# Feed-forward stages of an attention kernel: another order of the activations' low parts and the partial sums' copies on VectorE and ScalarE, one activation sum a step on GpSimd, last store in halves

## The chip, the cores and the metric

One core of a Trainium2 chip. The metric is the time of one execution on the device in microseconds (us), median of the runs. Engines by their short names: PE is TensorE, PEld its weight loads, DVE is VectorE, ACT is ScalarE, POOL is GpSimd, SP is SyncE (it only issues DMAs here).

## What is computed

```python
def reference(**kwargs):
    attn_out = _attn_ref(...)          # B, H, S, D = 4, 8, 576, 64: local softmax attention plus a memory read
    x = np.ascontiguousarray(attn_out.transpose(0, 2, 1, 3)).reshape(B * S, H * D)   # 2304 tokens x 512
    x = _moe_ref(x=x, **moe_kwargs)    # g = x @ w_gate; silu(g) * (x @ w_val) @ w_out      (512 -> 1536 -> 512)
    return _moe2_ref(x=x, **moe2_kwargs)   # h = x @ w_in; g = h where h >= 1, 0 where h <= -1, else (h + 1)**2 / 4; g @ w_out  (512 -> 2048 -> 512)
```

Everything is float32. The change touches only what follows the attention: the two feed-forward layers.

## The kernel before, in words

**Split numbers.** A float32 product is made of three fast matmuls: every operand is split into a high part (a copy rounded to the fast type, made by ACT) and a low part (raw minus high, made by DVE or POOL). `three` (lines 1284 to 1286) issues high x high, high x low, low x high.

**Steps.** The 2304 tokens are three superblocks (SB = 768, each held as two halves of 384 columns). Layer one takes 12 steps u for each superblock (u = 0 to 35, S1 = 12), layer two 8 steps (u = 36 to 59, S2 = 8). A step computes one tile of hidden units of the first layer or two of the second. The up projection of a step is a fast 2x2 scheme with seven products instead of eight: `product(u, n)`, n = 0 to 6, each of six matmuls of 384 columns. It needs seven forms of the activations, X0 to X6, for the superblock: four are the activations themselves or sums of them (X1, X3, X5, X6 are sums that POOL makes, `x_sum`, line 609), each with a high part by ACT (`x_high`, line 725) and a low part by DVE (`x_low`, line 972). There is one buffer for each of the seven, so the high part n of the next superblock waits until product n of the last step of this one has read it. Product n of the first step of a superblock waits for the low parts 0 to n. "Fresh" is the first step of a superblock (u = 12, 24, 36, 44, 52), "ends" the last (u = 11, 23, 35, 43, 51).

**Inside a step.** ACT copies partial sums out of PSUM: `copy_p1` (753) after product 0, `copy_p5` (758) after product 1, `copy_u2` (763) after product 3; product 3 waits for the first, product 4 for the second and product 5 for `copy_u2`, since they add onto the same banks. DVE adds them to further products: `c11` (1038), `c12` (1044), `c22` (1050); product 6 waits for `c22`. Layer one then has `silu` (ACT, 768) and `prod` (DVE, 1063), layer two `relu_half` (ACT, 793), `s_half` (DVE, 1073), `g_half` (DVE, 1079). The hidden tile gets its high part by `hid_high` (ACT, 778) and its low part by `hid_low` (DVE, 1067). Weights of the up projection for step u+1: high parts in three pieces by `up_high` (ACT, 706), low parts by `up_low` (POOL line 581, DVE line 963); piece 0 is POOL's always, at a change of superblock POOL has more of them. For the first superblock of each layer POOL also makes sums of the weights (562 to 571), which a DMA keeps in DRAM ("kept"); the low part waits until that DMA has read them.

**Down projection.** Two steps late (LAG = 2), in units: `down(n)`, six matmuls, into one of two banks, emptied by `add_down(n)` (DVE, line 1086 or 1089). Unit n waits for the add of unit n-2. A step has 4 units in layer one, 8 in layer two. After the last step 16 units are left (the tail), and then the last superblock's output goes out in four stores, one for each 128 rows (line 511).

**What sets the order.** No planner: each engine runs its own list, written out by hand in its block, and waits on semaphores. PE's list is fixed by `UP_ORDER` and by the places of the units, and the change leaves it alone. On ACT and DVE a step is a straight list of calls; whatever stands behind a waiting call waits too. POOL's list of a step is its low parts of the weights, the low parts of the down weights (line 587), the weight sums and the activation sums.

## Time and profile before

| | us |
|---|---|
| median of 3 runs (1024.37 to 1025.57) | 1025.43 |
| the profiled execution, its whole time | 1026.03 |
| its span in the trace | 1024.1 |
| PE busy / share | 987.5 / 96% |
| DVE busy / share | 805.0 / 79% |
| ACT busy / share | 565.0 / 55% |
| POOL busy / share | 506.4 / 49% |

The span is what the trace covers; 1.9 us of the whole time lie around it. In the trace a matmul's busy time is 0.33 us though the next one starts 0.17 us after it, so PE's busy share says little; what counts is where the next matmul starts late. Rows give times in us from the span's start, and in brackets the idle time of the engine before an instruction and who ended it.

### The profile page before, as it was taken

Reading aid. Unit: us, or ns where it says so; the run is one execution under the profiler, and the core shown is the slowest. Engines: PE = TensorE matmul, PEld = TensorE weight load, DVE = VectorE, ACT = ScalarE, POOL = GpSimd, SP = SyncE. Lnnn points to the kernel's source line nnn. Section 1 sums busy time; section 2 is a strip of 40 time slices with the busy share of each in tenths; the row PEclk is TensorE's granted clock in tenths of the full one; section 3 lists DMA queues with packets and bytes.
Section 4 is the critical chain, followed back from the end, with each engine's and each line's share of the span. In section 5 each row is a group of like instructions: output and inputs, shape, how many; then the busy total and the mean of one; then the engine's idle time right before and its main releaser. Section 6 shows DMA issues by size and latency. Waiting matters only on the chain.

```text
span 1024.1 us, 19136 instructions
## 1 busy us (share of the span) xinstructions
PE 987.5 (96%) x6328; PEld 918.4 (90%) x6328; DVE 805.0 (79%) x1422; ACT 565.0 (55%) x1130; POOL 506.4 (49%) x407
## 2 busy tenths in 40 slices
PE   6999999989999899998999999999999999999998
PEld 4766677789999899997999999999989999899997
DVE  6889999457778677676667778888898788978776
ACT  5888888564446444445454455454654546555541
POOL 5666777167567332274223376656643245432330
PEclk9999999999999999999999999999999999999999
DMA  6445443143443233332333223233232522225211
GB/s 226 134 145 185 143 144 121 52 144 118 120 147 105 89 117 104 104 112 73 104 135 112 103 84 124 68 118 125 82 107 80 186 83 104 84 102 185 69 36 62
DMA packets 34637, 116.13 MB, mean 113 GB/s; under 512 B 4208, under 2 KB 4336, under 8 KB 34544
## 3 DMA queue, kind: packets, MB, share of 16 engines
q1 hardware_dynamic: 34400, 114.91, 33.6%
q8 instruction: 55, 0.90, 0.4%
q14 instruction: 38, 0.31, 0.1%
q10 hardware_dynamic: 144, 0.00, 0.0%
HBM read 100.14 MB, written 14.75 MB: 112 GB/s over the span
## 4 chain that ended last, share of the span: by engine, by line
PE 85%; DVE 6%; issue 4%; ACT 2%; POOL 1%; DMA 0%; ACTq 0%; DVEq 0%; POOLq 0%
PE ps L1284 23%; PE ps L1286 22%; PE ps L1285 22%; PE ps L1241 6%; PE ps L1210 5%; PE ps L1267 5%; DVE xt_l L972 1%; DVE xy L1089 1%; DVE hid_r L1079 1%; DVE tmp L1073 1%; ACT wu_h L706 1%; PE ps L1222 1%; DVE hid_l L1067 1%; DVE hid_r L1063 0%; DMA qk<-qk_in 0%
## 5 line engine op out<-in xcount | busy, mean ns | idle before, releaser
L581 POOL TENSOR_TENSOR wu_l<-wu_r,wu_h 128x768 fp32r<-128x768 f32 (+1 forms) x75 | 140.1, 1875 | 404.1 <-ACT wu_h L706 404.1
L1284 PE MATMUL ps<-xt_h,wu_h 128*128 128x384 f32 x840 | 282.5, 336 | 15.6 <-DVE xt_l L972 9.9
L1286 PE MATMUL ps<-xt_h,wu_l 128*128 128x384 f32 x840 | 280.8, 334 | 0.0
L1285 PE MATMUL ps<-xt_l,wu_h 128*128 128x384 f32 x840 | 280.8, 334 | 0.0
L1284 PE MATMUL ps<-hid_h,wd_h 128*128 128x384 f32 x672 | 226.9, 338 | 8.0 <-DVE xy L1089 7.4
L1285 PE MATMUL ps<-hid_l,wd_h 128*128 128x384 f32 x672 | 225.3, 335 | 0.0
L1286 PE MATMUL ps<-hid_h,wd_l 128*128 128x384 f32 x672 | 225.2, 335 | 0.0
L1089 DVE TENSOR_TENSOR xy<-xy,ps 128x384 f32<-128x384 f32 x288 | 157.4, 548 | 56.3 <-PE ps L1286 55.4
L778 ACT ACTIVATE hid_h<-hid_r 128x768 fp32r<-128x768 f32 x84 | 70.9, 844 | 207.9 <-DVE hid_r L1063 148.1
L1284 PEld LDWEIGHTS ps<-xt_h,wu_h 128*128 128x128 f32 x840 | 157.6, 188 | 21.7 <-issue 21.6
L1285 PEld LDWEIGHTS ps<-xt_l,wu_h 128*128 128x128 f32 x840 | 157.7, 188 | 0.0
L1286 PEld LDWEIGHTS ps<-xt_h,wu_l 128*128 128x128 f32 x840 | 157.7, 188 | 0.0
L587 POOL TENSOR_TENSOR wd_l<-wd_r,wd_h 128x512 fp32r<-128x512 f32 x84 | 137.3, 1646 | 16.2 <-ACT wd_h L711 14.9
L1284 PEld LDWEIGHTS ps<-hid_h,wd_h 128*128 128x128 f32 x672 | 126.5, 188 | 14.0 <-issue 14.0
L963 DVE TENSOR_TENSOR wu_l<-wu_r,wu_h 128x512 fp32r<-128x512 f32 x105 | 121.4, 1157 | 6.8 <-DMA kept<-wu_r 3.8
L1285 PEld LDWEIGHTS ps<-hid_l,wd_h 128*128 128x128 f32 x672 | 126.7, 189 | 0.0
L1286 PEld LDWEIGHTS ps<-hid_h,wd_l 128*128 128x128 f32 x672 | 126.7, 189 | 0.0
L706 ACT ACTIVATE wu_h<-wu_r 128x512 fp32r<-128x512 f32 (+1 forms) x180 | 118.9, 693 | 0.0
L1067 DVE TENSOR_TENSOR hid_l<-hid_r,hid_h 128x768 fp32r<-128x768 f32 x84 | 82.9, 986 | 38.7 <-ACT hid_h L778 38.7
L676 ACT ACTIVATE rown<-negs,nmax 128x576 f32<-128x576 f32 (+3 forms) x128 | 77.2, 608 | 1.0 <-DVE nmax L905 1.0
L697 ACT ACTIVATE pt<-ps 128x512 f32<-128x512 f32 (+2 forms) x128 | 59.9, 494 | 29.4 <-PE ps L1241 29.1
L905 DVE CUSTOM_DVE_ANT_0 negs<-ps,mask 128x576 f32<-128x576 f32 (+3 forms) x128 | 65.7, 549 | 11.3 <-PE ps L1210 11.0
(84 smaller groups left out, 1342.4 us busy)
## 6 DMA issues: line engine op xcount, KB each, us to landing
wu_r<-w_up SPq DMA_DIRECT2D x60, 512.0 KB, 4.7
wd_r<-w_down SPq DMA_DIRECT2D x42, 512.0 KB, 3.7
wu_r<-kept SPq DMA_DIRECT2D x38, 512.0 KB, 5.7
kept<-wu_r SPq DMA_DIRECT2D x19, 512.0 KB, 4.6
qk<-qk_in SPq DMA_DIRECT2D x15, 640.0 KB, 4.8
nat<-nat_in SPq DMA_DIRECT2D x16, 384.0 KB, 5.4
vm<-vm_in SPq DMA_DIRECT2D x16, 320.0 KB, 2.9
rbc<-rsums SPq DMA_DIRECT2D x32, 144.0 KB, 3.0
```

The source lines that it names most:

```text
L581: nc.gpsimd.tensor_tensor(wu_l[u % 3][:, a:b], wu_r[u % 3][:, a:b], wu_h[u % 2][:, a - 1:b - 1].bitcast(F32), ALU.subtract).then_inc(low_p ...
L587: nc.gpsimd.tensor_tensor(wd_l[:, t % 6], wd_r[:, t % 6], wd_h[:, t % 6].bitcast(F32), ALU.subtract).then_inc(wd_lo, 1)
L676: nc.scalar.activation(head_rows(j)[:, h + (i == 1), D:D + w], negs[:, t % NEGS, 0:w], ACT.Exp, bias=nmax[:, p % 2, k:k + 1], scale=-1.0, ...
L706: nc.scalar.activation(wu_h[u % 2][:, a - 1:b - 1], wu_r[u % 3][:, a:b], ACT.Copy).then_inc(wu_hi[n], 1)
L778: nc.scalar.activation(hid_h[:, t % 6], hid_r[:, t % 6], ACT.Copy).then_inc(hh_done, 1)
L905: nc.vector.tensor_tensor_reduce(negs[:, t % NEGS, 0:w], psf[:, col:col + w], mask[:, S - w:S], -(float(D) ** -0.5), 3.0e38, ALU.add, ALU. ...
L963: nc.vector.tensor_tensor(wu_l[u % 3][:, a:b], wu_r[u % 3][:, a:b], wu_h[u % 2][:, a - 1:b - 1].bitcast(F32), ALU.subtract).then_inc(low_d ...
L1067: nc.vector.tensor_tensor(hid_l[:, t % 6], hid_r[:, t % 6], hid_h[:, t % 6].bitcast(F32), ALU.subtract).then_inc(hl_done, 1)
L1089: nc.vector.tensor_tensor(y, y, o, ALU.add).then_inc(evac, 1)
L1284: nc.tensor.matmul(dst, w_hi, v_hi, start=start, stop=False, skip_group_check=onto)
L1285: nc.tensor.matmul(dst, w_hi, v_lo, start=False, stop=False, skip_group_check=onto)
L1286: return nc.tensor.matmul(dst, w_lo, v_hi, start=False, stop=stop, skip_group_check=onto)
```

## The change

On **DVE**, layer one: at a fresh step X3's low part goes ahead of `hid_low`, X4's ahead of `c11`, X5's ahead of `up_low` piece 1 and `c12`, X6's ahead of `c22`; at a last step X0's and X1's low parts go behind `c12` and behind `c22` with its adds. Layer two: the first add of a fresh step goes ahead of X3's low part, X6's low part goes ahead of `c12`. The last `s_half` of all moves out of step 59 behind that step's last add, and the tail's adds and low parts are interleaved one place later.

On **ACT**, layer one: in steps 0 to 4 and at fresh and last steps `copy_u2` goes ahead of `down_high` and of `up_high` piece 2; at a fresh step X6's high part goes up to X5's. Layer two, fresh steps: `up_high` piece 0 goes up to piece 1, and both ahead of the `hid_high` that waits for `g_half`.

On **POOL** the four activation sums of the next superblock come one a step, five, four, three and two steps ahead, instead of two in each of the two steps before the last one.

On **SP** the last of the four final stores is split by columns: the first half goes after the last add but one, the second half after the last.

```diff
-            for c in range(CH):
+            for c in range(CH - 1):
                 at_least(sp, evac, UNITS * NGROUP - 2 * (CH - 1 - c))
...
-            sp.wait_ge(stored, 16 * (NSB - 1 + CH))
+            for t in range(2):
+                sp.wait_ge(evac, UNITS * NGROUP - 1 + t)
+                cols = slice(TOK - SB + HALF * t, TOK - SB + HALF * t + HALF)
+                sp.dma_start(out[(CH - 1) * P:, cols], xy[:, CH - 1, cols]).then_inc(stored, 16)
+            sp.wait_ge(stored, 16 * (NSB + CH))
...
@@ gpsimd
-                if u + 3 < STEPS and superblock(u + 3) != superblock(u + 2):
-                    x_sum(sb + 1, 1)
-                    x_sum(sb + 1, 3)
-                if u + 2 < STEPS and superblock(u + 2) != superblock(u + 1):
-                    x_sum(sb + 1, 5)
-                    x_sum(sb + 1, 6)
+                for n, ahead in ((1, 5), (3, 4), (5, 3), (6, 2)):
+                    if u + ahead < STEPS and superblock(u + ahead) != superblock(u + ahead - 1):
+                        x_sum(superblock(u + ahead), n)
...
@@ scalar, layer one
+                soon = u <= 2 * LAG or fresh or ends
...
                 if fresh:
                     x_high(sb, 5)
+                    x_high(sb, 6)
                 if ends:
                     x_high(sb + 1, 0)
                 if u > 0:
                     up_high(u + 1, 1)
                     up_high(u + 1, 0)
+                if soon:
+                    copy_u2(u)
                 for t in down_tiles(u):
                     down_high(t)
                 if u > 0:
                     up_high(u + 1, 2)
-                if fresh:
-                    x_high(sb, 6)
                 if ends:
                     x_high(sb + 1, 1)
-                copy_u2(u)
+                if not soon:
+                    copy_u2(u)
...
@@ scalar, layer two
-                if u > STEPS1:
+                if u > STEPS1 and not fresh:
                     hid_high(tiles_of(u)[0] - 1)
                 if more:
                     up_high(u + 1, 1)
+                if fresh:
+                    up_high(u + 1, 0)
+                    if u > STEPS1:
+                        hid_high(tiles_of(u)[0] - 1)
                 copy_p5(u)
...
@@ vector, layer one
+                if fresh:
+                    x_low(sb, 3)
                 if u > 2 * LAG:
                     hid_low(u - 1)
                 if fresh:
-                    x_low(sb, 3)
+                    x_low(sb, 4)
                 c11(u)
...
                 if fresh:
-                    x_low(sb, 4)
-                if ends:
-                    x_low(sb + 1, 0)
+                    x_low(sb, 5)
...
                 if fresh:
-                    x_low(sb, 5)
+                    x_low(sb, 6)
                 if ends:
-                    x_low(sb + 1, 1)
+                    x_low(sb + 1, 0)
                 c22(u)
                 for n in units[2:4]:
                     add_down(n)
-                if fresh:
-                    x_low(sb, 6)
+                if ends:
+                    x_low(sb + 1, 1)
                 prod(u, 1)
...
@@ vector, layer two
+                add_down(units[0])
                 if fresh:
                     x_low(sb, 3)
-                add_down(units[0])
...
+                if fresh:
+                    x_low(sb, 6)
                 c12(u)
                 add_down(units[4])
                 c22(u)
-                if fresh:
-                    x_low(sb, 6)
...
-                s_half(u, 1)
+                if more:
+                    s_half(u, 1)
                 add_down(units[7])
             tail = UNITS * (NGROUP - LAG)
+            s_half(STEPS - 1, 1)
+            add_down(tail)
             hid_low(2 * NGROUP - 2)
-            add_down(tail)
+            add_down(tail + 1)
             g_half(STEPS - 1, 1)
-            add_down(tail + 1)
             add_down(tail + 2)
+            add_down(tail + 3)
             hid_low(2 * NGROUP - 1)
-            for n in range(tail + 3, UNITS * NGROUP):
+            for n in range(tail + 4, UNITS * NGROUP):
                 add_down(n)
```

## Rows read from the trace of the kernel before

**Rows 1.** The page, part 1: busy time, share, instructions of each engine.
```profile
PE 987.5 (96%) x6328; PEld 918.4 (90%) x6328; DVE 805.0 (79%) x1422; ACT 565.0 (55%) x1130; POOL 506.4 (49%) x407
```

**Rows 2.** Who PE waited for, whole span: us in total, times, longest us.
```profile
PE ps L1284 <- DVE xt_l L972: 9.9, 8, 2.0
PE ps L1284 <- DVE xy L1089: 7.4, 14, 1.1
...
PE ps L1284 <- ACT u2s L763: 5.1, 5, 1.2
```

**Rows 3.** Timeline of PE, step 1: start us, us, what, idle before and releaser.
```profile
210.24 0.33 PE L1284 MATMUL ps<-xt_h,wu_h 128*128 128x384 f32 x1
...
211.11 0.34 PE L1286 MATMUL ps<-xt_h,wu_l 128*128 128x384 f32 x1
212.67 0.41 PE L1284 MATMUL ps<-xt_h,wu_h 128*128 128x384 f32 x1 [1.23 <-ACT u2s L763]
212.92 0.34 PE L1285 MATMUL ps<-xt_l,wu_h 128*128 128x384 f32 x1
```

**Rows 4.** Timeline of step 2: DVE's chain up to product 6 at 224.71.
```profile
221.16 1.23 DVE L963 TENSOR_TENSOR wu_l<-wu_r,wu_h 128x512 fp32r<-128x512 f32 x1 [1.50 <-DMA kept<-wu_r]
...
224.71 0.41 PE L1284 MATMUL ps<-xt_h,wu_h 128*128 128x384 f32 x1
```

**Rows 5.** Who PE waited for between 320 and 345 (first change of superblock).
```profile
PE ps L1284 <- DVE xt_l L972: 4.2, 3, 2.0
```

**Rows 6.** Timeline of step 12: DVE's way to the low part of X5, and PE.
```profile
333.66 0.56 DVE L1044 TENSOR_TENSOR hb<-u2s,ps 128x384 f32<-128x384 f32 x1 [1.40 <-ACT u2s L763]
...
334.78 1.24 DVE L972 TENSOR_TENSOR xt_l<-traw,xt_h 128x768 fp32r<-128x768 f32 x1
...
336.28 0.41 PE L1284 MATMUL ps<-xt_h,wu_h 128*128 128x384 f32 x1 [2.01 <-DVE xt_l L972]
```

**Rows 7.** Window: length, busy of PE, PEld, DVE, ACT, POOL, granted clock, DMA.
```profile
481.40:484.80 3.40, 3.40 (x13) 3.40 (x12) 1.11 (x2) 0.00 (x0) 0.00 (x0) 0.50 0.00 0
```

**Rows 8.** Who PE waited for between 605 and 645 (steps 35 to 37).
```profile
PE ps L1284 <- DVE xy L1089: 0.7, 2, 0.5
```

**Rows 9.** Timeline of steps 41 and 42: POOL's activation sums beside DVE's work.
```profile
710.63 1.86 POOL L609 TENSOR_TENSOR traw<-xy 128x768 f32<-128x768 f32 x1
711.09 2.22 DVE L1073 SCALAR_TENSOR_TENSOR tmp<-tmp 128x768 f32<-128x768 f32 x1 [1.25 <-ACT tmp L793]
...
712.64 2.37 POOL L609 TENSOR_TENSOR traw<-xy,traw 128x768 f32<-128x768 f32 x1
...
713.69 2.12 DVE L1067 TENSOR_TENSOR hid_l<-hid_r,hid_h 128x768 fp32r<-128x768 f32 x1
```

**Rows 10.** Who PE waited for between 710 and 735 (steps 42 and 43).
```profile
PE ps L1284 <- DVE xy L1089: 2.0, 4, 1.1
```

**Rows 11.** Who PE waited for between 838 and 862 (steps 49 to 51).
```profile
PE ps L1284 <- DVE xy L1089: 0.3, 2, 0.2
```

**Rows 12.** Who PE waited for between 745 and 765 (step 44, fresh).
```profile
PE ps L1284 <- DVE xy L1089: 1.7, 2, 1.0
PE ps L1284 <- DVE xt_l L972: 0.7, 1, 0.7
```

**Rows 13.** Timeline of step 44: DVE and ACT up to `hid_high`, then POOL's burst.
```profile
746.07 0.95 DVE L1073 SCALAR_TENSOR_TENSOR tmp<-tmp 128x768 f32<-128x768 f32 x1
...
749.25 0.85 ACT L778 ACTIVATE hid_h<-hid_r 128x768 fp32r<-128x768 f32 x1 [2.13 <-DVE hid_r L1079]
...
752.54 5.16 POOL L581 TENSOR_TENSOR wu_l<-wu_r,wu_h 128x768 fp32r<-128x768 f32 x3 [7.21 <-ACT wu_h L706]
753.61 1.68 DVE L972 TENSOR_TENSOR xt_l<-traw,xt_h 128x768 fp32r<-128x768 f32 x1
```

**Rows 14.** Timeline of PE in the tail.
```profile
1004.31 0.41 PE L1284 MATMUL ps<-hid_h,wd_h 128*128 128x384 f32 x1 [0.79 <-DVE xy L1089]
```

**Rows 15.** Window from the last store's issue to its landing, columns as in rows 7.
```profile
1021.40:1023.70 2.30, 0.00 (x0) 0.00 (x0) 0.00 (x0) 0.00 (x0) 0.00 (x0) 1.00 0.43 171
```

More of the change, by code:

```diff
@@ L850, in _ @@
                 if more:
-                    up_high(u + 1, 0)
+                    if not fresh:
+                        up_high(u + 1, 0)
                     up_high(u + 1, 2)
```

## Prediction

> **What bounds the kernel now.** I read the page first: PE is busy 96% of the span, DVE 79%, nobody else over 55% [rows 1]. So the end is PE's list, and only places where a matmul starts late can give time back. The second view is the list of waits on PE [rows 2]: low parts of activations 9.9 us in 8 waits, adds of partial sums 7.4 in 14, `copy_u2` 5.1 in 5. The timeline shows what such a wait costs: in steady flow a matmul starts every 0.174 us (210.24 to 211.11 is five starts); the stalled one starts 1.56 after the one before, so 1.39 is lost where 1.23 is printed, and the next is 0.08 late too [rows 3]. **Each printed wait costs its time plus 0.24 us.** That makes 12, 11 and 6 us, about 29 in all, plus some 5 us of stalls too short to be printed. This is all that the reordering can win, apart from the clock and the end. The third view is the same list for each stretch where the change acts; the rows before a stall on DVE tell who held its queue.
>
> **copy_u2, steps 1 to 3.** Three waits of 1.23, so 4.4 us. Moving the copy ahead of `down_high` and `up_high` piece 2 gives back about 1 us of each at product 5. But product 6 of step 2 starts at 224.71 because DVE's chain has just ended there: it started at 221.16, when the DMA "kept" had read the weight sums that POOL makes, 1.50 us of DVE idle before it [rows 4]. POOL's sums of steps 1 to 3 are not moved, so this chain ends when it did, and the same holds one and two steps later. PE gets to product 5 earlier and waits at product 6 instead. I cost this edit at **0**; bounds 0 to 4.4.
>
> **Changes of superblock in layer one (12, 24).** Product 3 to 6 of the fresh step wait 4.2 us in 3 printed waits, and twice more below the print, with restarts 5.3 [rows 5]; step 24 has the same rows. At step 12 the low part of X5 (334.78) stands behind `c12`, which sits idle 1.40 for `copy_u2`, which stands on ACT behind five other copies; product 5 then starts at 336.28 after 2.01 idle [rows 6]. X6's stands behind `c22` and two adds, which themselves wait for PE. In the new order none of the four stands behind a wait of that kind. The walk, with t = 0 where product 2 starts, 1.04 us (six starts) for each product or unit on PE, 0.95 for a low part, 0.85 for a high part [rows 13], 0.56 for an add or a copy [rows 6], and 0.25 from a low part's end to PE (334.78 + 1.24 to 336.28 is 0.26) [rows 6]. PE wants product 3 at 2.1 (a unit lies between), 4 at 3.2, 5 at 5.3 and 6 at 8.4. DVE: X2 ends just before 0, `prod` 0.3, X3 1.2, then it waits for `hid_high` (to 1.1), `hid_low` 2.1, X4 3.25, so product 4 starts at 3.5, 0.3 late; `c11` 3.75, add 4.25, X5 5.2, in time for product 5 at 5.6; but ACT has `copy_u2` behind five copies and reaches it at 5.7, 0.25 late. `up_low` 5.9, `c12` and add to 7.0, X6 beside POOL up to 8.7, `c22` 9.2, product 6 about 0.3 late. X2 itself is 0.3 late. With a restart for each 1.3 us remain. Gain 4.0 each, **8.0** for both (6 to 9). Moving X0 and X1 of the last step behind `c12` and `c22` costs nothing: product 1 comes 2 us after product 0's turn, and X1 is ready 0.1 before it; if that cover is gone it costs what X1 is late. It does free `c12` and the add behind it at step 11: **0.6**.
>
> **copy_u2 at steps 23 and 35.** The two other waits of [rows 2]: 5.1 less three of 1.23 is 1.4, with restarts **1.9**, all gone, for `c12` isn't otherwise late there.
>
> **The clock.** From 481.4 to 484.8 the granted clock is 0.50, 1.2 GHz [rows 7], right behind step 24's stall of 2.0 us at product 5, and matmuls start 0.32 apart instead of 0.17: 1.6 us lost. The equal stall of step 12 did not do this. With the stall down to 0.3 I expect the fall gone: **1.6** (0 or 1.6).
>
> **Step 36.** Adds hold PE 0.7 us in 2 waits, 1.2 with restarts [rows 8]. The first add goes ahead of X3, but behind `hid_low` of step 35, and that chain now starts no earlier, while PE is about 1 us earlier: **0.3** (-0.5 to 1.2).
>
> **Activation sums.** POOL's sums take 1.86 and 2.37; the DVE instructions beside them take 2.22 and 2.12 [rows 9] where 0.95 and 0.94 are usual [rows 13]. Two sums in a row cost DVE 2.4 us, more than its slack of about 0.9 in a layer-two step, and PE stalls: 2.0 in 4 waits at steps 42 and 43, 3.0 with restarts [rows 10]; 0.3 in 2 waits at 49 to 51, 0.8 with restarts [rows 11] and as much below the print. One sum a step costs about 1.2 in each of four steps, which is nearly slack: I leave 0.2 to 0.3 of stall in each. Gain **1.5** and **0.8** (0 to 3.5 together), and 0.3 for the same at steps 21 and 33.
> The Trainium skill ("SBUF — State Buffer", Who interferes with whom) says that a DVE instruction with two SBUF inputs contends with a GpSimd instruction that reads SBUF, and that one with a single SBUF input does not. This trace agrees: the adds, with one input in PSUM, stay at 0.54 in all of it.
>
> **Fresh steps of layer two (44, 52).** Each stalls 2.4 us in 3 waits, 3.1 with restarts [rows 12]. ACT stands idle 2.13 for `g_half` [rows 13]; the new order puts the two `up_high` there. So POOL's burst of three weight low parts, 5.16 us, starts not at 752.54 but as soon as they are done, about 748.5. There DVE has `g_half`, X3, `hid_low` and X4, all of two SBUF inputs; a low part beside POOL took 1.68 [rows 13]. The burst leaves the late ones and lands on the early ones, on which products 3 and 4 wait. Walking it with such work at half speed beside POOL (0.95 by 1.68): `g_half` ends at 749.9 and the add that unit 194 needs at 750.4, 0.1 sooner than now; X3 ends at 752.2 and product 3 starts at 752.45, 0.6 later than it does; `hid_low` ends at 754.0, X4 at 756.1, product 4 is 2.4 later. From there POOL is done sooner, X6 and `s_half` run alone, and most of it comes back: step 45 starts 0.45 later than now. **-0.9** for both; bounds -4 (each of four instructions loses 1.2 where now three do) to +5 (the stalls go).
>
> **Tail and last store.** Unit 321 waits 0.79, cost 1.03 [rows 14], because its add is behind the last `s_half`, which waits for ACT; now it goes first, and no other unit gets later by more than 0.1: **1.0** (0.7 to 1.4). The last store moves packets for 0.43 of 2.30 us, so 0.99 [rows 15]; half as much data after the last add saves **0.5** (0 to 1.0; the issue of 0.33 of the first half is over before).
> The skill ("DMA: Bandwidth & Descriptors", Rules for kernel authors) speaks against it: small transfers should be merged, since they are mostly fixed cost. Its fit in the Anatomy section, 2.0 us and bytes / 436e9 (for another issue path), would make half of 384 KB worth 0.45 us, by estimate; the fixed cost of the first half lies beside the last add, so the rule does not bite.
>
> **Sum.** 8.0 + 0.6 + 1.9 + 1.6 + 0.3 + 1.5 + 0.8 + 0.3 - 0.9 + 1.0 + 0.5 = 15.6 us. Span 1024.1 to 1008.5, profiled execution 1026.03 to 1010.4. The median of the runs was 0.6 under the profiled one, so 1009.8.
>
> **Rivals.**
> *Layer two gains too.* ACT's idle time is the real limit at 44 and 52 and POOL's earlier burst is spread harmlessly: of 2 x 3.1 us most goes instead of 0.9 lost. 5 to 6 us better, 1004.5. For it: ACT idles 2.13. Against: DVE has no idle time there.
> *Layer two gives back.* DVE is the bound in steps 36 to 59; the sums merely shift the loss (no gain of 2.3) and the burst costs 2 us at each fresh step: 1015.
> *The stalls of layer one only move.* As in steps 1 to 3, another chain (X2, `copy_p1`, `hid_low`) stands right behind at 12 and 24, so that 8.0 is 2 and the clock still falls: 1018 to 1020.
> *Slower.* One place: POOL against DVE in steps 39 to 42 and 47 to 52. If a single sum costs DVE 2.4 us as two do now, each of eight steps stalls by that less the slack of 0.9, 12 us, and the fresh steps lose 4: 16 us against 15.6 gained elsewhere and here. It decides only from about 2.4 us for each sum; a sum alone has about half of that by [rows 9].
> *It does not do what it says*: the waits name other releasers than the order; within 0.2%.
>
> **Chances.** Forecast (1006.5 to 1013) 0.55; layer two gains too 0.18; gives back 0.16; stalls only move 0.06; no change 0.03; slower 0.02. A measurement of this kernel can tell about 0.2%, 2 us, from nothing. The range leaves out the slowest cases and half of the fastest: 1004 to 1016. Faster by over 0.2% 0.95, within 0.03, slower 0.02.
>
> **What would show it.** Right: PE's waits for low parts fall from 9.9 to about 2 us; no row with clock 0.50 after 21 us; `copy_u2` gone from the waits after step 3 but product 6 of step 2 still 13.6 us after 211.11; DVE instructions beside POOL at 44 take 1.7 to 2 on X3 and `hid_low`. Wrong: if steps 1 to 3 get shorter than 8.9 us each, if step 44 loses its stalls, or if units 160 to 175 (steps 39 to 41) stall by more than 0.3 each.

## The result, and the profile after

The changed kernel takes 1014.5 us (median of 4 runs, 1013.51 to 1016.36), the kernel before in the same comparison 1025.5 (1024.37 to 1025.79): ratio 0.9897, 95% interval 0.9879 to 0.9915. That is 11.0 us faster where 15.6 were forecast, inside the stated range (1004 to 1016) but above its inner part (1006.5 to 1013). The profiled execution took 1013.51 with a span of 1011.6, so between the two profiled executions 12.5 us lie. The two differ because the changed kernel's profiled execution was the fastest of its four, 1.0 us under their median, and the one before was 0.5 above its own. The tables below are all from profiled executions, so their gains add up to 12.5 within 0.2.

The page's first part and who PE waited for (us in total, times, longest us), to be read against [rows 1, 2]:

```profile
PE 987.5 (98%) x6328; PEld 916.8 (91%) x6328; DVE 813.9 (80%) x1422; ACT 564.0 (56%) x1130; POOL 503.7 (50%) x407
...
PE ps L1296 <- DVE xy L1098: 5.6, 10, 1.0
PE ps L1296 <- DVE xt_l L981: 2.8, 5, 0.9
...
PE ps L1296 <- DVE hb L1059: 0.9, 2, 0.4
PE ps L1296 <- POOL wu_l L585: 0.7, 3, 0.3
PE ps L1296 <- ACT u2s L764: 0.6, 3, 0.2
```

Waits for low parts fell from 9.9 to 2.8 us and those for `copy_u2` from 5.1 to 0.6; waits for adds only from 7.4 to 5.6, and two new names appear: `c22` (L1059) and POOL's low parts of the weights (L585). DVE has the same 1422 instructions and is busy 8.9 us longer. The experiments below show DVE instructions getting longer where they lie beside POOL.

To see where the rest went I added up, for each step, how much later than 0.1733 us after its forerunner each matmul starts. This "lost" time includes the small stalls that the list of waits leaves out, and is in us. Wherever the text below says what a step loses, it means this.

| steps | lost before | lost after | gain | forecast |
|---|---|---|---|---|
| 1 to 4 | 5.4 | 4.4 | 1.0 | 0 |
| 11, 12 | 6.3 | 0.8 | 5.5 | 4.6 |
| 24 (with the clock) | 7.0 | 0.7 | 6.2 | 5.6 |
| 23, 35 | 1.9 | 0.5 | 1.4 | 1.9 |
| 36, 37 | 1.7 | 2.6 | -1.0 | 0.3 |
| 19 to 21, 31 to 33 | 0.6 | 1.9 | -1.3 | 0.3 |
| 40 to 43 | 3.0 | 3.0 | 0.0 | 1.5 |
| 47 to 51 | 1.5 | 1.4 | 0.1 | 0.8 |
| 44, 52 | 6.4 | 7.2 | -0.8 | -0.9 |
| tail | 1.9 | 0.9 | 1.0 | 1.0 |
| last matmul's start to the end | 3.7 | 3.2 | 0.5 | 0.5 |

**Step 12**, DVE's timeline, against [rows 6]:

```profile
330.20 0.95 DVE L981 TENSOR_TENSOR xt_l<-traw,xt_h 128x768 fp32r<-128x768 f32 x1
331.07 0.68 DVE L972 TENSOR_TENSOR wu_l<-wu_r,wu_h 128x512 fp32r<-128x512 f32 x1
331.87 0.55 DVE L1053 TENSOR_TENSOR hb<-u2s,ps 128x384 f32<-128x384 f32 x1
332.34 0.55 DVE L1098 TENSOR_TENSOR xy<-xy,ps 128x384 f32<-128x384 f32 x1
332.81 1.47 DVE L981 TENSOR_TENSOR xt_l<-traw,xt_h 128x768 fp32r<-128x768 f32 x1
```

X5's low part is done at 331.15, ahead of `c12` (L1053); product 5 starts at 331.98, 0.18 late for `copy_u2`. X6's (332.81) is ready before it is wanted. Nothing of this stretch is left in the list of waits.

**Step 44**, DVE's and POOL's timeline, against [rows 13]:

```profile
736.29 0.94 DVE L1088 TENSOR_TENSOR hid_r<-hb,tmp 128x768 f32<-128x768 f32 x1
737.15 0.54 DVE L1098 TENSOR_TENSOR xy<-xy,ps 128x384 f32<-128x384 f32 x1
737.62 2.15 DVE L981 TENSOR_TENSOR xt_l<-traw,xt_h 128x768 fp32r<-128x768 f32 x1
739.69 2.04 DVE L1076 TENSOR_TENSOR hid_l<-hid_r,hid_h 128x768 fp32r<-128x768 f32 x1
741.64 0.54 DVE L1098 TENSOR_TENSOR xy<-xy,ps 128x384 f32<-128x384 f32 x1
742.11 1.56 DVE L981 TENSOR_TENSOR xt_l<-xy,xt_h 128x768 fp32r<-128x768 f32 x1
...
736.64 6.22 POOL L585 TENSOR_TENSOR wu_l<-wu_r,wu_h 128x768 fp32r<-128x768 f32 x3 [4.63 <-ACT wu_h L707]
```

POOL's burst starts 0.35 us into `g_half`, which keeps its 0.94. The next three DVE instructions with both inputs in SBUF take 5.75 us together where they would take 2.85 (three times 0.95); the two adds with an input in PSUM stay at 0.54. Who PE waited for there (735 to 752), against [rows 12]:

```profile
PE ps L1296 <- DVE xy L1098: 1.3, 2, 1.0
PE ps L1296 <- DVE xt_l L981: 1.1, 2, 0.8
```

**The last store**: the window from the second half's issue to its landing, against [rows 15]. It is 1.9 us long instead of 2.3, and packets move for 0.49 of it, 0.93 us. That is hardly less than the 0.99 of the whole store, but the end of the first half's packets lies in it too: they move until 1009.7, the second half's from 1010.0 to 1010.8.

```profile
1009.30:1011.20 1.90, 0.00 (x0) 0.00 (x0) 0.00 (x0) 0.00 (x0) 0.00 (x0) 0.90 0.49 177
```

### The profile page after: what moved, and what is told of

The parts are those of the page before. It is cut to its first block, busy times and chain, and to the rows that moved or that the text cites. A ratio compares the mean times of both kernels' runs of the same rounds, so it can differ in the third digit from the quotient of the medians.

```text
span 1011.6 us, 19137 instructions
## 1 busy us (share of the span) xinstructions
PE 987.5 (98%) x6328; PEld 916.8 (91%) x6328; DVE 813.9 (80%) x1422; ACT 564.0 (56%) x1130; POOL 503.7 (50%) x407
## 4 chain that ended last, share of the span: by engine, by line
PE 88%; DVE 5%; issue 3%; ACT 2%; DMA 1%; POOL 1%; DVEq 0%; ACTq 0%; POOLq 0%
PE ps L1296 24%; PE ps L1297 23%; PE ps L1298 23%; PE ps L1253 6%; PE ps L1222 5%; PE ps L1279 5%; DVE xt_l L981 1%; DVE xy L1098 1%; DVE hid_l L1076 1%; PE ps L1234 1%; DVE hid_r L1088 1%; DMA qk<-qk_in 0%; PE ps L1274 0%; ACT tmp L794 0%; DVE negs L914 0%
## 5 line engine op out<-in xcount | busy, mean ns | idle before, releaser
L585 POOL TENSOR_TENSOR wu_l<-wu_r,wu_h 128x768 fp32r<-128x768 f32 (+1 forms) x75 | 142.2, 1904 | 398.8 <-ACT wu_h L707 398.8
L591 POOL TENSOR_TENSOR wd_l<-wd_r,wd_h 128x512 fp32r<-128x512 f32 x84 | 136.6, 1639 | 15.1 <-ACT wd_h L712 13.9
L1076 DVE TENSOR_TENSOR hid_l<-hid_r,hid_h 128x768 fp32r<-128x768 f32 x84 | 85.4, 1016 | 36.9 <-ACT hid_h L779 36.9
L914 DVE CUSTOM_DVE_ANT_0 negs<-ps,mask 128x576 f32<-128x576 f32 (+3 forms) x128 | 65.8, 550 | 12.5 <-PE ps L1222 12.2
```

The costliest lines, as they stand in the source:

```text
L585: nc.gpsimd.tensor_tensor(wu_l[u % 3][:, a:b], wu_r[u % 3][:, a:b], wu_h[u % 2][:, a - 1:b - 1].bitcast(F32), ALU.subtract).then_inc(low_p ...
L591: nc.gpsimd.tensor_tensor(wd_l[:, t % 6], wd_r[:, t % 6], wd_h[:, t % 6].bitcast(F32), ALU.subtract).then_inc(wd_lo, 1)
L914: nc.vector.tensor_tensor_reduce(negs[:, t % NEGS, 0:w], psf[:, col:col + w], mask[:, S - w:S], -(float(D) ** -0.5), 3.0e38, ALU.add, ALU. ...
L1076: nc.vector.tensor_tensor(hid_l[:, t % 6], hid_r[:, t % 6], hid_h[:, t % 6].bitcast(F32), ALU.subtract).then_inc(hl_done, 1)
```

## The experiments

The theories from the profile of the changed kernel were three: (A) an activation sum on POOL costs DVE about its own length wherever it lies beside two-input work, so spreading the sums buys nothing; (B) at steps 44 and 52 the edit on ACT, the early burst, is what costs, and DVE's edit would win alone; (C) step 36 is late because X0's and X1's low parts were moved back in step 35. Against each stands that DVE simply has too much to do there.

### e1_old_sums

```diff
-                for n, ahead in ((1, 5), (3, 4), (5, 3), (6, 2)):
-                    if u + ahead < STEPS and superblock(u + ahead) != superblock(u + ahead - 1):
-                        x_sum(superblock(u + ahead), n)
+                if u + 3 < STEPS and superblock(u + 3) != superblock(u + 2):
+                    x_sum(sb + 1, 1)
+                    x_sum(sb + 1, 3)
+                if u + 2 < STEPS and superblock(u + 2) != superblock(u + 1):
+                    x_sum(sb + 1, 5)
+                    x_sum(sb + 1, 6)
```

> The changed kernel with one part undone: POOL's activation sums two in each of the two steps before the last, as before. In the changed kernel steps 19, 20, 31, 32 each lose 0.3 us on PE that they did not lose before, and steps 40 to 43 and 47 to 51 lose 3.0 and 1.4 us, as much as before (3.0 and 1.5). Theory A (a sum beside DVE costs DVE about the same whether it comes alone or second in a row, so spreading brings nothing in layer two and costs layer one 1.2 us): PE's lost time falls by 1.0 to 1.5 us against the changed kernel, all of it at steps 19, 20, 31, 32; steps 40 to 43 stay within 0.7 of 3.0. Theory B (spreading does gain its 2.3 us as predicted, and something else in the change takes it away again): steps 40 to 43 and 47 to 51 get slower by 2 us or more than in the changed kernel, and the whole by 1 us or more.

Measured: 1014.2 us, ratio to the kernel before 0.9887 (0.9871 to 0.9904), which can't be told from the changed kernel's. Its profile says more: steps 19, 20, 31 and 32 lose nothing (1.3 us back), steps 40 to 43 lose 3.0 and 47 to 51 1.5, the same as with the sums spread. Step 4 lost 1.7 in this profile against 0.5, which hides the gain in the total. Theory A holds as far as it goes: spreading brought nothing in layer two and cost 1.3 us in layer one. In layer one the moment at which the sum runs is at fault. DVE and POOL at step 19 of the changed kernel, start and length:

```profile
412.81 2.05 DVE L972 TENSOR_TENSOR wu_l<-wu_r,wu_h 128x512 fp32r<-128x512 f32 x1
414.79 0.54 DVE L1059 TENSOR_TENSOR hb<-p5s,ps 128x384 f32<-128x384 f32 x1
...
412.47 1.84 POOL L613 TENSOR_TENSOR traw<-xy 128x768 f32<-128x768 f32 x1
```

The low part of a weight piece, 0.68 alone (step 12 above), takes 2.05 beside the sum, and `c22`, on which product 6 waits, stands behind it.

### e2_tiny_sums

```diff
+                dst = raw_sum(sb, n)
+                if sb > 1:
+                    a, b, dst = a[:, :, 0:8], b[:, :, 0:8], dst[:, :, 0:8]
-                nc.gpsimd.tensor_tensor(raw_sum(sb, n), a, b, ALU.subtract).then_inc(tp, 1)
+                nc.gpsimd.tensor_tensor(dst, a, b, ALU.subtract).then_inc(tp, 1)
```

> The changed kernel with the activation sums for superblocks 2 to 5 cut to 8 of 384 columns of each half, so POOL works on them for a moment only; the waits stay. What is left out is most of those sums, so the output is not the reference's. If the sums' collision with DVE is the cause of the stalls of steps 19 to 21, 31 to 33, 40 to 43 and 47 to 51 (1.9 + 3.0 + 1.4 = 6.2 us lost on PE in the changed kernel), under 1 us of them is left, and nothing changes at steps 36, 44 and 52. If those steps are simply too long for DVE without any collision, more than half stays.

This leaves out most of the sums, so the output is not the reference's.

Measured: one run, 1007.4 us. All the steps named lose 0.0; steps 44 and 52 lose 3.6 each (3.4 and 3.7 in the changed kernel), step 36 2.3 instead of 2.6. So the sums on POOL are the whole of those 6.3 us. The rows of e1 show how they act, by the DVE instructions beside them.

### e3_late_burst

```diff
-                if u > STEPS1 and not fresh:
+                if u > STEPS1:
                     hid_high(tiles_of(u)[0] - 1)
...
-                if fresh:
-                    up_high(u + 1, 0)
-                    if u > STEPS1:
-                        hid_high(tiles_of(u)[0] - 1)
                 copy_p5(u)
...
-                    if not fresh:
-                        up_high(u + 1, 0)
+                    up_high(u + 1, 0)
```

> The changed kernel with one part undone: at steps 36, 44 and 52 ACT does hid_high before the up_high pieces again and piece 0 after copy_p5, so POOL's burst of weight low parts starts about 4 us later, as before. DVE's order stays the new one. Theory of the prediction (the early burst lands on X3, hid_low and X4, on which products 3 and 4 wait, and the stalls there are its price): the stalls at product 3 and unit 195 of step 44 go (2.1 us of 3.4), others come back behind, and step 44 loses 2.5 to 3.3 us instead of 3.4, step 52 likewise. Rival (DVE has too much to do in these steps wherever the burst lies, and the early start of up_high is worth something in itself): step 44 loses 3.4 us or more.

Measured: one run, 1010.0 us, faster than any of the changed kernel's. Steps 44 and 52 lose 1.8 and 2.0 instead of 3.4 and 3.7. Both expectations missed, on the same side: I had taken the burst for a shift of the loss, and it was half of it. (Step 42 loses 1.4 instead of 1.9 as well; why is open.) DVE's and POOL's timeline at step 44:

```profile
737.47 0.95 DVE L976 TENSOR_TENSOR xt_l<-traw,xt_h 128x768 fp32r<-128x768 f32 x1
738.34 0.94 DVE L1071 TENSOR_TENSOR hid_l<-hid_r,hid_h 128x768 fp32r<-128x768 f32 x1
739.21 0.54 DVE L1093 TENSOR_TENSOR xy<-xy,ps 128x384 f32<-128x384 f32 x1
739.67 0.95 DVE L976 TENSOR_TENSOR xt_l<-xy,xt_h 128x768 fp32r<-128x768 f32 x1
...
740.41 5.85 POOL L585 TENSOR_TENSOR wu_l<-wu_r,wu_h 128x768 fp32r<-128x768 f32 x3 [8.54 <-ACT wu_h L707]
```

With the burst late, X3, `hid_low` and X4 keep their 0.95, and the burst falls beside six DVE instructions that read PSUM and only two that don't, X5 and X6.

### e4_step35_old

```diff
+                if ends and u == STEPS1 - 1:
+                    x_low(sb + 1, 0)
                 if u > 0 and 1 not in pieces_of_pool(u):
                     up_low(u + 1, 1)
                 c12(u)
...
                 if ends:
-                    x_low(sb + 1, 0)
+                    x_low(sb + 1, 1 if u == STEPS1 - 1 else 0)
                 c22(u)
...
-                if ends:
+                if ends and u < STEPS1 - 1:
                     x_low(sb + 1, 1)
```

> The changed kernel with one part undone at step 35 alone: the low part of X0 goes ahead of up_low piece 1 and c12 again, and X1's ahead of c22. In the changed kernel step 36 loses 2.6 us on PE where it lost 1.4 before; unit 130 alone 1.1, behind hid_low 35, which waits for hid_high 35 and prod. Theory A (X0 and X1 moved back at step 35 make prod, hid_high and hid_low 35 late, and through them the first adds of step 36): step 36 loses 1.0 to 1.8 us; step 35 may lose up to 1 us more. Theory B (step 36 is late because DVE's own order in it and POOL's earlier burst are the bound): step 36 still loses 2.3 us or more.

Measured: one run, 1012.0 us; step 36 loses 1.4 instead of 2.6, step 35 nothing instead of 0.25. Theory A of this run holds. PE starts step 35 at 590.73 in the changed kernel and at 590.84 here, so the times of the two can be compared as they stand. The changed kernel's DVE before unit 130, and PE at it:

```profile
604.25 1.49 DVE L981 TENSOR_TENSOR xt_l<-xy,xt_h 128x768 fp32r<-128x768 f32 x1
605.66 0.54 DVE L1072 TENSOR_TENSOR hid_r<-hb,ps 128x384 f32<-128x384 f32 x1
607.17 0.96 DVE L1076 TENSOR_TENSOR hid_l<-hid_r,hid_h 128x768 fp32r<-128x768 f32 x1 [0.96 <-ACT hid_h L779]
608.04 0.55 DVE L1098 TENSOR_TENSOR xy<-xy,ps 128x384 f32<-128x384 f32 x1
...
608.74 0.41 PE L1296 MATMUL ps<-hid_h,wd_h 128*128 128x384 f32 x1 [0.96 <-DVE xy L1098]
```

`prod` ends at 606.20, ACT's high part follows, DVE idles 0.96, then `hid_low`, then the add PE wants for unit 130, which costs 1.2 us. In this experiment `prod` starts at 604.04, 1.6 earlier, and the unit costs 0.3:

```profile
602.62 1.49 DVE L981 TENSOR_TENSOR xt_l<-xy,xt_h 128x768 fp32r<-128x768 f32 x1
604.04 0.54 DVE L1072 TENSOR_TENSOR hid_r<-hb,ps 128x384 f32<-128x384 f32 x1
```

### e5_only_u2

The kernel before with the `soon` edit of `copy_u2` alone:

```diff
+                soon = u <= 2 * LAG or fresh or ends
...
+                if soon:
+                    copy_u2(u)
                 for t in down_tiles(u):
                     down_high(t)
...
-                copy_u2(u)
+                if not soon:
+                    copy_u2(u)
```

> The kernel before with one part of the change alone: copy_u2 ahead of down_high and up_high piece 2 in steps 0 to 4 and at the fresh and last steps of layer one. Theory of the prediction (in steps 1 to 4 the gain at product 5 is taken back at product 6, which waits for DVE's chain behind the DMA that keeps the weight sums): steps 1 to 4 lose 5.3 us on PE together as before, within 0.3 but for step 4, where that DMA's own time moves the wait by 0.8; steps 23 and 35 lose 0.9 us less each; steps 12 and 24 win under 1 us, since X5 and X6 still stand behind c12 and c22. In all 2 to 3 us faster. Rival (the copy alone was what held step 12 too: X5's low part waited behind c12, and c12 for the copy): steps 12 and 24 win 1.5 us or more each, in all 4 us or more.

Measured: one run, 1023.5 us. Steps 1 to 4 lose 5.0 (5.4 before); 23 and 35 nothing, 1.9 us back; step 12 still 5.4; step 24 loses 5.9, 0.4 more than in e8 and e10 below (5.5), where the clock did not fall at it either; step 36 loses 2.2, 0.7 more. This is the prediction's side: moving the copy alone brings nothing at 12 and 24. Of the 2.5 us between this profile and the one before, 1.6 are the clock fall that did not come here, so the copy's own worth is 0.9. That step 36 loses more because PE gets there earlier is argued, not shown.

### e6_timed_sums

```diff
+                for n, ahead in ((1, 5), (3, 4), (5, 3), (6, 2)):
+                    if u + ahead < STEPS and superblock(u + ahead) != superblock(u + ahead - 1):
+                        if u < STEPS1:
+                            pool.wait_ge(hl_done, u)
+                        else:
+                            pool.wait_ge(g_done, 2 * (u - STEPS1))
+                        x_sum(superblock(u + ahead), n)
                 for n in pieces_of_pool(u):
```

> The changed kernel with the activation sums in the same steps, but at the head of POOL's list of the step and held until DVE has something else to do: in layer one until hid_low of the step is done, in layer two until the step before's second g_half is. Cutting the sums took away all the loss at steps 19 to 21, 31 to 33, 40 to 43 and 47 to 51, so where they fall beside DVE should decide. If what costs is the overlap with DVE instructions that have two inputs in SBUF: in layer one the sum lies beside c11 and an add, and the six steps lose under 0.4 us instead of 1.9; in layer two it lies beside hid_low 0.45 us after DVE's idle time and the steps lose under 1.5 us instead of 4.4. If a sum costs DVE the same wherever it lies: 1.5 and 4 us or more stay.

Measured: one run, 1013.3 us. Layer one as hoped: the six steps lose 0.0 instead of 1.9. Layer two the other way: steps 39 to 43 lose 2.8 and 47 to 51 2.5, 5.3 together instead of 4.4. My reading of DVE's idle 0.45 us was wrong as to its worth. DVE and POOL at step 39, which loses 1.0 here and nothing in the changed kernel:

```profile
655.53 1.83 DVE L1080 TENSOR_TENSOR hid_l<-hid_r,hid_h 128x768 fp32r<-128x768 f32 x1 [0.45 <-ACT hid_h L783]
657.74 1.93 DVE L976 TENSOR_TENSOR wu_l<-wu_r,wu_h 128x512 fp32r<-128x512 f32 x1
...
654.69 1.85 POOL L613 TENSOR_TENSOR traw<-xy 128x768 f32<-128x768 f32 x1 [3.65 <-DVE hid_r L1092]
657.27 1.85 POOL L585 TENSOR_TENSOR wu_l<-wu_r,wu_h 128x768 fp32r<-128x768 f32 x1 [0.73 <-ACT wu_h L711]
```

The sum lengthens `hid_low` by 0.9, and that delay pushes DVE's low part of a weight piece behind the start of POOL's own, where it takes 1.93 instead of 0.68. So place decides in layer one, where DVE has several idle stretches in a step; in layer two no place on POOL that I tried was free.

### e7_best

The edits of e3, e4 and e6 together.

> The changed kernel with three things put right together: ACT's order at fresh steps of layer two as before (won 3.4 us), X0's and X1's low parts at step 35 as before (won 1.5 us), the sums timed as in the run before this one. If the three are independent: PE loses about 23.6 - 3.4 - 1.5 - 4.5 = 14 us in the feed-forward part, and the time is about 1004 us, 0.990 of the changed kernel and 0.979 of the one before. If they overlap (the stalls they free are taken up by the next one in DVE's list): 1007 us or more.

Measured: 1007.8 us, ratio 0.9829 (0.9812 to 0.9845); 17.4 us lost on PE. Missed by 3 to 4 us, and past the 1007 that was set for parts that overlap. The figures say otherwise: I had counted 4.5 for the timed sums, and layer two gave -0.9. The rest adds up: 23.6 - 3.4 (44, 52) - 1.9 (19 to 33) - 1.7 (36) + 0.9 = 17.5. So the three parts do not get in each other's way.

### e8_tail_store

The kernel before with the diff's tail and last store alone.

> The kernel before with two parts of the change alone: the tail's new order (last s_half behind the last add of step 59, adds one place earlier) and the last store in halves. Prediction's terms: 1.0 us less lost on PE in the tail (1.9 to 0.9), and 0.5 us less from the last matmul's start to the end of the span (3.68 to 3.2 us); nothing else moves. If the half store had to wait for the other half, or a smaller store took as long as a whole one, the second stays at 3.6 or more.

Measured: the tail loses 0.86 instead of 1.88, and 3.21 us instead of 3.68 lie between the last matmul's start and the end. Both terms as forecast. The time, 1024.8 in one run, says nothing, for in this profile the clock fell once, at step 12 (6.9 us lost there) and not at step 24 (5.5).

### e9_dve_sums

e7 with layer two's sums on DVE:

```diff
...
+                    if u < STEPS1 and superblock(u + ahead) != superblock(u + ahead - 1):
+                        pool.wait_ge(hl_done, u)
+                        x_sum(superblock(u + ahead), n)
...
                 c11(u)
                 add_down(units[2])
+                for n, ahead in ((1, 5), (3, 4), (5, 3), (6, 2)):
+                    if u + ahead < STEPS and superblock(u + ahead) != superblock(u + ahead - 1):
+                        x_sum_dve(superblock(u + ahead), n)
```

> The last version (fresh steps' ACT order and step 35 as before, sums of layer one timed beside c11) with the activation sums of layer two taken from POOL to DVE itself, behind c11 and its add, where DVE is idle 0.84 us before it can do the next add. Moving the sum on POOL to another moment made layer two worse (5.7 us lost at steps 39 to 42 and 47 to 50 against 4.4), so a sum that lies beside DVE's two-input work costs DVE about as long as the sum takes. If that is the cost, a sum of 0.95 us on DVE in an idle slot is cheaper than one of 1.9 on POOL: those eight steps lose under 1 us, and the time is 1003 us (0.978 of the kernel before). If DVE simply has no room for more in layer two, they lose 3 us or more and the time is 1006 or more.

Measured: 1003.6 us (1003.20 to 1006.68), ratio 0.9796 (0.9776 to 0.9817). Steps 39 to 51 but 44 lose 0.1 us together. DVE at step 40, and POOL beside it, start and length:

```profile
672.28 0.55 DVE L1109 TENSOR_TENSOR xy<-xy,ps 128x384 f32<-128x384 f32 x1
672.75 1.68 DVE L1099 TENSOR_TENSOR traw<-xy,traw 128x768 f32<-128x768 f32 x1
674.35 0.55 DVE L1109 TENSOR_TENSOR xy<-xy,ps 128x384 f32<-128x384 f32 x1
674.81 1.32 DVE L968 TENSOR_TENSOR wu_l<-wu_r,wu_h 128x512 fp32r<-128x512 f32 x1
...
671.37 2.24 POOL L585 TENSOR_TENSOR wu_l<-wu_r,wu_h 128x768 fp32r<-128x768 f32 x1 [5.71 <-ACT wu_h L708]
```

The sum takes 1.68 and not the 0.95 that I had counted, since POOL's low part lies beside it, and still costs PE nothing: half of it (0.84) lies where DVE waited for the next unit, and behind it stand only things with slack. This version is 1.1% faster than the changed kernel (1003.55 to 1014.53).

### e10_only_burst

The kernel before with the change's ACT order at steps 36, 44 and 52 alone (the `fresh` lines that e3 takes out).

> The kernel before with one part of the change alone: ACT's order at steps 36, 44 and 52 (up_high pieces 1 and 0 ahead of the hid_high that waits for g_half), so POOL's burst starts 4 us earlier. Undoing it in the changed kernel won 1.7 us at each of steps 44 and 52. If the early burst is harmful in itself, steps 44 and 52 lose 3.8 to 5 us each here instead of 3.2. If it is harmful only together with DVE's new order (first add ahead of X3), they lose 3.2 or less.

Measured: one run, 1027.7 us; steps 44 and 52 lose 4.3 and 4.1. As measured that is the first answer, the burst harmful in itself. PE waits once, 2.3 us, where three stalls of about 1 us stood before, and behind that wait, or inside it, the clock fell in both steps. Here is one of the windows (columns as in [rows 7]):

```profile
752.50:755.90 3.40, 3.40 (x13) 3.40 (x12) 3.40 (x5) 0.18 (x1) 1.95 (x1) 0.50 0.00 0
```

Each fall costs about 1.6 us, as in [rows 7], and 2.7 and 2.5 are left, less than the 3.2 before. With e3 this makes a square of what step 44 and step 52 lose:

| | DVE's old order | DVE's new order |
|---|---|---|
| ACT's old order | 3.2, 3.2 | 1.8, 2.0 |
| ACT's new order | 4.3, 4.1 (2.7, 2.5 with the clock taken out) | 3.4, 3.7 |

DVE's edit alone helps. ACT's alone shortens the stalls by 0.6 a step but gathers them into one, and with the clock falls it costs 1.0; one run can't say how often they would come. Both together hurt. The early burst stretches X3 with either order of DVE (2.15 in the changed kernel, 2.58 here), and DVE's gain shows only where the burst is late:

```profile
748.78 2.58 DVE L977 TENSOR_TENSOR xt_l<-traw,xt_h 128x768 fp32r<-128x768 f32 x1
```

### e11_l1_low_only

The kernel before with layer one's DVE order and X6's high part alone, `copy_u2` where it was.

> The kernel before with the low parts of layer one alone in the new order (DVE's order at fresh and last steps, X6's high part moved up), copy_u2 where it was. copy_u2 alone won nothing at step 12 (5.4 us lost) and 1.1 at step 24. Prediction: the low parts are what product 3 to 6 wait for, and 4 of 5.4 us are theirs; with copy_u2 still last in ACT's list product 5 then waits for it: steps 12 and 24 lose 1.5 to 2.5 us each instead of 0.8, and step 11 0.8 or more. Rival: the low parts gain only once copy_u2 is early, since c12 stands ahead of X6: 3.5 us or more stay at each.

Measured: one run, 1019.9 us. Steps 12 and 24 lose 1.8 and 1.9: the low parts alone bring 3.6 of the 4.6. Step 11 loses 0.2, not 0.8. At step 36 the moved low parts show their price: 4.6 us where 1.4 stood, of which 1.6 are a clock fall behind a start 2.1 late.

## Why the prediction was right where it was, and wrong where it wasn't

**The account as a whole.** Each printed wait was to cost its time and 0.24 us. At step 44 of the changed kernel four waits of 2.4 us are printed, which makes 3.4, and 3.4 are lost. Between the profiles 12.5 us came of 15.6. The missing 3.1 are the difference of misses with both signs: the activation sums 3.8 and step 36 1.3 too little, steps 23 and 35 0.5 too little, steps 1 to 4 1.0, steps 11 and 12 0.9 and step 24 0.6 too much. So the total is nearer than its parts, and that is luck.

**Layer one's fresh steps: right in mechanism, a little small.** Forecast to keep 1.3 us, step 12 keeps 0.8: 0.2 at product 2, 0.3 at product 4, 0.3 at product 5 for the copy, as the walk had it; product 6, 0.3 late in the walk, was not late at all. e11 and e5 show that the low parts carried it (3.6 of 4.6 us), that the copy did nothing alone, and that it brings the last 1.0 once the low parts are early.

**copy_u2 in steps 1 to 4: near the forecast 0, and the mechanism right from step 2 on.** The pair of profiles shows 1.0. The same order lost 5.0 to 5.5 us in e1 to e6 and in e9, and 4.4 in the changed kernel and e7, 5.0 in the mean; the old order lost 5.4 to 5.6 in the kernel before, e8, e10 and e11, 5.5 in the mean. Step 1 gains 1.0 in all of them, which the forecast had at nothing. Steps 2 and 3 gain nothing: product 5 loses 0.5 instead of 1.5, and the new waits for POOL's low part at product 0 and for `c22` at product 6 (the two new names on the list of waits) take up the rest. Step 4 then loses anything from 0.5 to 1.7, where the old order lost 0.6 to 0.9. Why it varies is open. The chain at step 2, against [rows 4]:

```profile
221.42 0.75 DVE L972 TENSOR_TENSOR wu_l<-wu_r,wu_h 128x512 fp32r<-128x512 f32 x1 [2.02 <-DMA kept<-wu_r]
...
224.49 0.41 PE L1296 MATMUL ps<-xt_h,wu_h 128*128 128x384 f32 x1 [0.43 <-DVE hb L1059]
```

The DVE chain now starts at 221.42 and product 6 at 224.49. That is 13.2 us after the last start before product 5 of step 1 (211.29), 0.4 sooner than the 13.6 that the prediction named as a sign.

**The clock: right for the profiles.** In the feed-forward part the clock fell in no profile without a start late by over 2 us. In the kernel before, e5, e8, e10 and e11 there are 11 such starts, 2.1 to 2.5 us late, and 6 of them had a fall: five within 1.4 us behind the start, one from 0.3 before it, inside the wait. So the 1.6 us were never certain to be lost before (e5 has the same stalls and no fall). And two of the changed kernel's four timed runs, at a mean clock of 0.996, took 1.8 and 2.9 us more than its profiled one at 1.000. Where they lost it no profile shows; that stays open.

**Activation sums: wrong, by 3.8 us, the largest miss.** The step that failed is "one sum a step costs about 1.2 in each of four steps, which is nearly slack". Forecast 2.6 (1.5 + 0.8 + 0.3), measured -1.2. Two things were wrong in it. In layer two I took 1.2 as the price of one sum and DVE's slack of 0.9 as free for it. The price is not fixed. By the rows in the last section it is what is left of POOL's sum when the DVE instruction starts, less 0.13, so up to 1.7 for a sum of 1.84. In the changed kernel an `s_half` beside one sum takes 2.67 where 0.95 is usual:

```profile
700.40 2.67 DVE L1082 SCALAR_TENSOR_TENSOR tmp<-tmp 128x768 f32<-128x768 f32 x1 [0.79 <-ACT tmp L794]
...
700.41 1.84 POOL L613 TENSOR_TENSOR traw<-xy 128x768 f32<-128x768 f32 x1
```

And the stall came in eight steps (40 to 42 and 47 to 51) instead of five. Steps 40 and 41 lose 0.6 and 0.5, which was one of the prediction's own signs of being wrong. In layer one I counted a gain at 21 and 33 and forgot the four new places, 19, 20, 31 and 32, at which a single sum meets the same low part; the row to read was `up_low` beside the sum at step 21. e2 shows that the sums on POOL are all of it, e1 that the old places were no worse in layer two, e6 and e9 where the sums do fit. (In the rival "slower" the prediction set 16 us against 15.6 gained. That sum is off: the 15.6 still held the sums' own 2.6 and the -0.9 of the fresh steps, and 13.9 were forecast elsewhere.)

**Step 36: wrong, 1.3 us.** "Moving X0 and X1 of the last step costs nothing" was argued for product 1 alone. The step that failed is the cover: behind X1 in DVE's list stand `prod`, and through ACT `hid_high`, `hid_low` and the first adds. At steps 12 and 24 the first unit stands behind product 2. At step 36 one stands behind product 0 already and then behind every product, so the adds are wanted sooner. e4 gives 1.3 us back at step 36 and 0.25 at step 35.

**Steps 44 and 52: right in sign, size and mechanism as a whole** (-0.8 by -0.9; X3 2.15, `hid_low` 2.04, X4 1.56 where the walk leaves 1.8, 1.8 and 1.6). Unit 194, which the walk let wait almost as before, lost nothing where it had lost 0.9, and the waits behind it made up for that. The parts were not weighed one by one: the DVE edit alone would have won 2.6 us (e3), which also refutes that the place of the burst only shifts the loss.

**Tail and store: right**, 1.0 and 0.5, and e8 shows them alone.

Of the rivals the one named "layer two gives back", at 1015, lies 0.5 us from the median, nearer than the forecast's 1009.8. It is right through one of its two causes, the sums, and wrong in the other: the burst cost 0.4 at each fresh step and not 2.

## What to carry to other kernels

When one engine slows another, moving work between moments is no gain in itself: list which instructions of the one lie beside it, and place it beside those that aren't touched (here the ones with an input in PSUM), or give it to the engine that is hindered, in a slot where that one waits anyway. Two reorderings can spoil each other when one decides when a burst comes and the other who stands in its way, so try such edits in a square of four, not as one; and count one long stall as dearer than several short ones of the same sum where the clock can fall behind it. And when a step of one instruction is moved back, follow everything behind it in that engine's list up to the next point where the bounding engine waits, in the densest stretch that uses the same code.

## What the runs showed of the hardware

A DVE instruction with both inputs in SBUF that starts while a POOL instruction is running ends a fixed time after that one ends, whenever it started. For 768 columns that is 0.82 us: 700.40 + 2.67 against 700.41 + 1.84, 711.09 + 2.22 against 710.63 + 1.86 [rows 9], and 672.75 + 1.68 against 671.37 + 2.24 in e9. In the feed-forward part of the changed kernel all 48 such DVE instructions of 768 columns ended 0.81 or 0.82 us behind POOL's, and all 63 low parts of 512 columns 0.55 behind it. Alone the two sizes take 0.95 and 0.68. So DVE does not run slowly beside POOL: it waits for POOL's end and then needs 0.13 us less than alone, at either size. DVE's adds and copies with one input in PSUM took 0.54 to 0.56 throughout.

This agrees with the exclusive lock that the Trainium skill ("SBUF — State Buffer", Who interferes with whom) describes for the read interface that the two share. It speaks against the half speed that I used in the walk.

In the feed-forward part a granted clock of 0.50 lasted 3.4 us each time and cost 1.4 to 1.6 us on PE. It came only with a start 2.1 us or more late, and there in 6 of 11 cases, three of them in e10 (steps 12, 44 and 52).
